# Taking the idle-time transpositions of TensorE out of the routing stage

## The reference, cut to what matters

```python
# layer 1, for each block of the sequence
intra = einsum('bhij,bhjd->bhid', einsum('bhic,bhjc->bhij', qb, kb) * Dmask, vb)
out[:, :, sl] = intra + einsum('bhid,bhde->bhie', qb * lam_pow, kv_state)
# layer 2, for each token s of a sequence
fresh_e = argmax(logits[b, s])               # logits = x @ w_gate
e = fresh_e if s == 0 or local_gate[b, s] < 0.5 else prev_e
out[b, s] = softmax(logits[b, s])[e] * (maximum(x[b, s] @ w1[e], 0) @ w2[e])
# layer 3
k = maximum(xk @ w_k, 0);  v = k * k @ w_v;  out = sigmoid(xr @ w_r) * v
```

## Time and profile before

| | us |
|---|---|
| runs of the kernel before | 495.94, 496.53, 497.08 |
| their median | 496.53 |
| the profiled execution's own time | 496.07 |
| its span, first to last instruction | 494.3 |
| mean granted clock of TensorE | 0.971 |

### The profile page before, as it was taken

How to read it: one execution, slowest core, us unless ns; L and a number is a source line. 1 busy time by engine, 2 the same in 40 slices (tenths; PEclk the granted TensorE clock), 3 DMA queues, 4 the chain that set the end, 5 groups by cost and what they waited for, 6 DMA issues and landing times.

```text
span 494.3 us, 7689 instructions
## 1 busy us (share of the span) xinstructions
PE 458.2 (93%) x2635; PEld 390.7 (79%) x2636; DVE 260.5 (53%) x421; ACT 210.9 (43%) x337; POOL 92.7 (19%) x137
## 2 busy tenths in 40 slices
PE   5399999589999999999999998399999999999997
PEld 5388888478887877887878786289889889889985
DVE  2268696529192828373746465496454534525401
ACT  0114333036372737282828283386444633615400
POOL 2215872532222222222122221100000000000000
PEclk9599999899999999999999999799999999999999
DMA  5899994027475655556585710610010000010001
GB/s 108 257 406 374 350 346 184 2 66 249 177 228 198 225 201 198 207 206 218 181 328 171 253 42 23 214 62 1 21 45 0 21 21 21 0 42 21 0 23 42
DMA packets 28552, 70.86 MB, mean 143 GB/s; under 512 B 3248, under 2 KB 4272, under 8 KB 28528
## 3 DMA queue, kind: packets, MB, share of 16 engines
q1 hardware_dynamic: 22992, 57.94, 33.7%
q0 software_dynamic: 2800, 9.18, 5.5%
q10 hardware_dynamic: 2736, 3.43, 2.1%
HBM read 59.01 MB, written 11.01 MB: 142 GB/s over the span
## 4 chain that ended last, share of the span: by engine, by line
PE 80%; DVE 8%; DMA 3%; issue 3%; SPq 2%; POOL 1%; DVEq 1%; ACT 0%; POOLq 0%; ACTq 0%
PE bank L1023 21%; PE bank L1025 20%; PE bank L1024 20%; DVE wl L789 5%; PE bank L953 3%; PE bank L929 3%; PE bank L942 2%; PE bank L963 2%; PE bank L1047 2%; PE bank L971 2%; DMA qk_sb<-in_qk_dram 2%; PE bank L1033 2%; POOL slot_row L405 1%; PE bank L917 1%; PE bank L978 1%
## 5 line engine op out<-in xcount | busy, mean ns | idle before, releaser
L789 DVE TENSOR_TENSOR wl<-raw,wh 128x1024 fp32r<-128x1024 f32 x64 | 74.6, 1218 | 0.0
L508 ACT ACTIVATE wh<-raw 128x1024 fp32r<-128x1024 f32 x64 | 64.0, 1052 | 0.0
L783 DVE TENSOR_TENSOR hl<-bank,hh 128x512 fp32r<-128x512 f32 x32 | 22.1, 690 | 64.1 <-ACT hh L504 64.1
L1023 PE MATMUL bank<-wh,hh 128*128 128x512 f32 x128 | 52.7, 412 | 2.6 <-DVE hl L783 1.6
L1023 PE MATMUL bank<-wh,xh 128*128 128x512 f32 x128 | 51.4, 402 | 1.7 <-DVE xl L779 1.7
L1025 PE MATMUL bank<-wh,hl 128*128 128x512 f32 x128 | 50.1, 391 | 0.0
L1025 PE MATMUL bank<-wh,xl 128*128 128x512 f32 x128 | 50.0, 391 | 0.0
L1024 PE MATMUL bank<-wl,hh 128*128 128x512 f32 x128 | 50.0, 390 | 0.0
L1024 PE MATMUL bank<-wl,xh 128*128 128x512 f32 x128 | 49.8, 389 | 0.0
L499 ACT ACTIVATE h_sb<-bank 128x512 f32<-128x512 f32 x32 | 19.1, 596 | 64.6 <-PE bank L1025 64.6
L1023 PE MATMUL bank<-xkh,wh 128*128 128x384 f32 x128 | 43.1, 336 | 1.1 <-DVE xkl L855 1.1
(11 more groups left out here) (159 smaller groups left out, 892.7 us busy)
## 6 DMA issues: line engine op xcount, KB each, us to landing
raw<-in_w_dram SPq DMA_DIRECT2D x64, 512.0 KB, 8.4
qk_sb<-in_qk_dram SPq DMA_DIRECT2D x12, 512.0 KB, 7.8
kv_sb<-in_kv_dram SPq DMA_DIRECT2D x12, 512.0 KB, 6.7
x_dram<-keep ACTq DMA_DIRECT2D x12, 256.0 KB, 5.9
keep<-y_dram SPq DMA_DIRECT2D x12, 256.0 KB, 5.1
out_dram<-o_sb SPq DMA_DIRECT2D x12, 256.0 KB, 2.0
raw<-in_w_k_dram SPq DMA_DIRECT2D x4, 512.0 KB
raw<-in_w_v_dram SPq DMA_DIRECT2D x4, 512.0 KB
```

Of the source, the lines that this page charges most:

```text
L508: act.activation(parts[1 - p][0][:, c, :], raw[:, c, :], ACT.Copy).then_inc(s["part_h"], 1)
L783: dve.tensor_tensor(hl[:, 4 * g:4 * g + 4, :], by(psT[g][:, :], 4), hh[:, 4 * g:4 * g + 4, :].bitcast(F32), ALU.subtract).then_inc(s["hl_d ...
L789: dve.tensor_tensor(parts[1 - p][1][:, c, :], raw[:, c, :], parts[1 - p][0][:, c, :].bitcast(F32), ALU.subtract).then_inc(s["part_l"], 1)
L1023: pe.matmul(ps, lhsT=a_high, rhs=b_high, start=start, stop=False)
```

## The change

The four groups of the routing stage are taken out; those of the first microseconds stay, and nothing else is edited.

```diff
             pe.wait_ge(s["keep_done"], FIRST + NT)
-            keep_warm(10, psO)
             pe.wait_ge(s["code_done"], 1)
             pe.transpose(psX[0:NT, 0:P], code[:, :], ident[:, :]).then_inc(s["code_ps"], 1)
             pe.wait_ge(s["run_done"], 1)
             pe.transpose(psL[:, 0:NT], runT[:, :], ident[0:NT, 0:NT]).then_inc(s["run_ps"], 1)
             pe.matmul(psU[:, 0:NT], lhsT=runT[:, P - 1:P].to_broadcast([NT, P]), rhs=ident[0:NT, 0:NT],
                       start=True, stop=True).then_inc(s["run_ps"], 1)
-            keep_warm(8, psO)
             pe.wait_ge(s["onehot_done"], 1)
...
             pe.matmul(psK[:, 0:E], lhsT=ones[:, :], rhs=upto[:, NT - 1:E * NT:NT], start=True, stop=True).then_inc(s["place_ps"], 1)
-            keep_warm(12, psO)
             for n in range(NT):
...
-            keep_warm(30, psO)
             x_tile_transposes(0)
             pe.wait_ge(s["plan_done"], 1)
```

## The result

| | before | after |
|---|---|---|
| median of 6 runs, us | 496.63 | 498.38 |
| lowest and highest | 495.94 to 497.08 | 497.63 to 499.04 |
| the profiled execution's own time | 496.07 | 497.63 |
| its span | 494.3 | 495.8 |
| mean granted clock | 0.971 | 0.955 |

The ratio is 1.0036, with a 95% interval of 1.0022 to 1.005: 1.8 us slower, and clear of no change. The forecast was 498.3.

The account below looks back on a forecast made before the run. From 104.69 us to the end of the experts TensorE's own products were taken as the bound. Terms -0.5 + 0.1 + 0 + 0.4 + 2.2 = +2.2 us on the profiled 496.07 gave 498.3, range 496.8 to 499.6.

Parts of the forecast that it names:

- The 4.88 us of the chain are not to be had: Group of 30 before the `x_tok` transpositions: gather ends together with it, so removal frees 0 to 0.4 us, taken as 0.
- The first products at half clock, +2.2 us: First expert products without the 30: half clock until it returns, losing half that time, 2.2 us as middle of bounds.
- The `x_tok` transpositions, +0.4 us: Four `x_tok` transpositions before the first expert product: at half clock 1.05 us instead of 0.62, 0.4 us lost.
- The group of 10, -0.5 us: Routing stage, transposition of `code`: without the 10 in front it starts 0.52 us sooner, at 85.71.
- The small matmuls at half clock, +0.1 us: Routing stage before the gather: clock falls sooner, perhaps at 87 to 91, so small matmuls lose 0 to 0.2, taken 0.1.
- the 0.46: Profiled execution, 496.07 us, lay 0.46 us below the median 496.53; the sum was counted from its own time.
- The early return: Rival at the first expert products: clock returns early, products lose 0.2 us, 496.3 to 497.0, no change; chance 0.11.
- The faster rival: Rival before the `x_tok` transpositions: the 30 end last, not the gather; four start 0.4 us sooner, 495.7; chance 0.05.
- That the 30 bring nothing: Rival at the first products: the 30 don't bring the clock back, half-clock start already before, 495.7; chance 0.02.
- The much slower case: Rival in the first tile: 8 to 10 us of half clock, costing 4 to 5 us, 500 to 501; chance 0.07.

Follow-up runs that it names:

- e1: Kernel before with only the group of 30 taken out, the groups of 10, 8 and 12 kept: 498.51 us, ratio 1.0053.
- e4: Kernel before with the group of 30 made 45: 497.78 us, ratio 1.0034.
- e8: Kernel before with 72 identity transpositions added in the idle time before the last layer: 496.2 us, ratio 1.0.
- e2: Kernel before with the groups of 10, 8 and 12 taken out and the 30 kept: 495.71 us, ratio 0.9992.
- e12: e7 with the groups of 10, 8, 12 and 30 all taken out: 496.46 us, ratio 0.9999 to the kernel before.
- e10: e7 with the groups of 10, 8 and 12 taken out and the 30 kept: 494.45 us, ratio 0.9963 to the kernel before.
- e6: Kernel before with all four routing groups out and two identity transpositions behind each of the 12 slot products: 498.76 us, ratio 1.0048.
- e3: Kernel before with the group of 30 made 20: 496.2 us, ratio 1.0016.
- e7: Kernel before with 104 instead of 24 identity transpositions behind the first scores of the attention: 494.67 us, ratio 0.9968.
- e5: Kernel before without groups of 10, 8 and 12, with two transpositions behind each slot product, the 30 kept: 497.66 us, ratio 1.0024.

## Why the prediction was right

*The 4.88 us of the chain are not to be had.* Shown for the execution that the forecast read. The gather is right behind: 3.47 us from its issue to the `x_tok` transpositions before, 3.42 after, 3.46 in e1. e4 shows the other side: a longer group is on the path at once. Where the clock returns late, some of the 30 are a delay after all, of 1.0 to 1.2 us (e8, e2), which the forecast had at nothing.

*The first products at half clock, +2.2 us.* Shown, in size too. The first tile took 2.25 us more for 4.7 us of half clock, 2.4 more for 5.1 in e1, and 2.6 more for 5.6 in e12, where it took 15.35 us. Each is 0.47 to 0.48 of the time, a little under the half that the forecast took. The forecast had no row for the return here and took the middle between returns after 3.0 and 5.8 us, so that 2.2 and 2.25 lie so close is partly luck. Putting the 30 back is worth 2.0 us (e12 to e10), and taking only them out costs 2.5 (e1). Nothing hides it: from the second tile to the start of the last expert product it is 189.97 us after, against 189.98.

*The `x_tok` transpositions, +0.4 us.* 2.30 us before, 2.76 after, from their start to the first product: +0.46.

*The group of 10, -0.5 us.* 0.88 to 0.52 us from `code` to the scan after, and to 0.46 in e2: -0.4. The transposition did not start 0.05 us after `code` but 0.14.

*The small matmuls at half clock, +0.1 us.* Too small by a factor of three. From the scan to `tile_max` it is 0.95 before and 1.21 after, and 0.03 more to `slot_row`: +0.29. The clock fell at 84.8 and not at 87 to 91, so all of them ran at half clock. And I had priced them by one 96-column matmul each (0.04 us), while the L1002 and L1003 chain (three with their weight loads) takes 0.72 us instead of 0.47. So the gain of the first group is nearly used up by the time the gather is issued, where the forecast kept 0.4 us of it. The longer `x_tok` transpositions are no longer cancelled, and the first product comes 0.35 us later after `code` than before, where the forecast had no difference.

*The sum.* Terms as measured: -0.36 (group of 10) + 0.29 (small matmuls) - 0.05 (gather) + 0.46 (`x_tok` transpositions) + 2.25 (products) = +2.6 us, against +2.2 predicted. The mechanism holds and the small terms were sized too low.

The medians differ by 1.8 us, 0.8 less than these terms. The forecast reached 1.8 by taking 0.46 off, since it thought that the profiled execution had an early return of the clock and so lay below its median. The early return is borne out: where the clock returns late, the 30 last 6.1 to 6.3 us and delay the path by 1.0 to 1.2 (e8, e2), and with no group there the changed kernel can't pay this. But the same profiled execution had a late return in the attention, and `code` was ready 1.1 us later in it than in the changed kernel's profile, which the forecast did not consider. The two nearly cancel, so the 0.46 is not explained by the first alone. How often the kernel before has each kind isn't known, and the 0.8 us is accounted for by argument only. That 498.3 met 498.38 to a tenth is luck; that the change costs about 2 us, and by what, is not.

*The rivals.* The early return did not occur in any of the four executions that were profiled without warming right in front of the products (the changed kernel, e1, e6, e12): 4.7 to 5.6 us each. The faster rival fell with the landing, which still came 3.4 us after the gather's issue when nothing stood in front of the transpositions. That the 30 bring nothing is refuted by e12 against e10. The Trainium skill's rule behind that rival ("TensorE: Matmul & The Clock Gate", Part 4: PE-mode transpose) is one with which these runs disagree: by it the clock would not rise for transpositions, and in the kernel before it rose at 100.8 after nothing but them since 97.47. The much slower case did occur, but at the last layer, and not in this change: the 12 us of e3.

## What to carry to other kernels

The largest piece of a chain can end at the same moment as something that runs beside it. Look for what would end last without it before counting it as a gain.

Work that keeps TensorE's clock up paid here where it reached to the start of the dense work. 30 transpositions right in front of it were worth 2.0 to 2.5 us, and 80 more in front of the attention 1.6 us. 24 spread over the slot products, with 4.5 us idle behind them, were worth nothing (e6). In front of a stretch in which TensorE waits for other engines it gained nothing (e8). A group in front of a small step on the path is a delay, and it grows when the clock is down: the 10 took 1.31 us at full clock and 2.25 at half (e7). So the small groups are the part of this change that could go: without them the time was the same or slightly lower (e2, e10).

## What the runs showed of the hardware that I had not expected

- The same instructions got the full clock back at 25.7 us in one execution and at 23.3 in another, with TensorE's start at 19.86 and 19.84. The products after the idle routing stage had it 4.7 to 5.6 us after the first of them. The moment isn't fixed by the program: the difference of 2.4 us in the attention made `code` 1.1 us later.
- The clock stayed at half for 12 us at the start of the last layer (e3), with TensorE busy for 10.7 of them: transpositions with waits of 0.15 to 0.65 us between, and 3.7 us of dense products at the end. It cost 3.05 us. In e5 it was 9.0 us, of which TensorE was busy for 7.9, and cost 1.2.
- The clock fell at 83.2 in e7, 0.9 us after the end of a stretch in which TensorE had been busy without a pause from 20.48 to 82.31.
- Two small changes of the warming (e3, e5) gave runs in two clusters 2 to 3 us apart, where the kernel before has one. The median over such clusters depends on how many runs fall in each: 7 of 12 in the lower one in e3, 3 of 12 in e5.
